# Two products in place of three for the experts' half-filled last tile, and a program whose arms hold the rest of each stretch

## What is computed

```python
for e in range(E):                      # 8 experts
    for k in range(2):                  # first and second choice
        mask = top2[:, k] == e
        h = np.maximum(x[mask] @ w1[e], 0.0)          # 512 -> 1024
        out[mask] += top2_w[mask, k, None] * (h @ w2[e])   # 1024 -> 512
```

## Time and profile before

| what | us |
|---|---|
| median of three runs | 1034.64 (1032.08 to 1034.65) |
| the profiled execution | 1032.71 |
| its span, first to last instruction | 1030.7 |
| TensorE busy in it | 1014.0 (98%) |
| mean granted clock of TensorE | 0.995 of full speed |

### The profile page before, as it was taken

One profiled execution on the slowest core, in us unless ns is written; L12 is line 12 of the kernel. 1 busy time (PEld: TensorE's weight loads), 2 busy tenths in 40 slices (PEclk: granted clock), 3 DMA queues, 4 the chain that ended last, 5 costly groups with the idle time before them and its releaser, 6 DMA issues.

```text
span 1030.7 us, 16726 instructions
## 1 busy us (share of the span) xinstructions
PE 1014.0 (98%) x5934; PEld 932.6 (90%) x5935; DVE 446.0 (43%) x935; ACT 370.1 (36%) x683; POOL 529.8 (51%) x416
## 2 busy tenths in 40 slices
PE   7999999999999999999999999999999999999997
PEld 6999999888989898989898998989898989899895
DVE  6888888773214232433325652222222222222221
ACT  6998988853213132322223413212121212111110
POOL 8698999520000202020202136978788887878752
PEclk8999999999999999999999999999999999999999
DMA  8788886383960101010402175262717163634304
GB/s 175 176 198 200 208 209 164 96 274 116 369 247 1 62 0 62 0 62 0 143 1 73 52 233 167 91 175 71 186 40 212 22 194 71 187 78 140 44 2 51
DMA packets 73986, 124.97 MB, mean 121 GB/s; under 512 B 13377, under 2 KB 30913, under 8 KB 73938
## 3 DMA queue, kind: packets, MB, share of 16 engines
q1 hardware_dynamic: 65218, 104.05, 34.1%
q0 software_dynamic: 8640, 20.00, 9.7%
q10 hardware_dynamic: 80, 0.29, 0.1%
HBM read 78.73 MB, written 36.67 MB: 112 GB/s over the span
## 4 chain that ended last, share of the span: by engine, by line
PE 75%; DVE 1%; issue 0%; POOL 0%; ACT 0%; DVEq 0%; POOLq 0%
PE ps_turn L1714 13%; PE ps_x L1690 10%; PE ps_b L1690 10%; PE ps_x L1779 10%; PE ps_a L1761 9%; PE ps_b L1761 9%; PE ps_small L1714 9%; PE ps_a L1670 2%; PE ps_small L1662 1%; PE ps_turn L1652 1%; PE ps_small L1644 0%; POOL out L1274 0%; PE ps_turn L1802 0%; PE ps_small L1645 0%; DVE y_tile L1455 0%
## 5 line engine op out<-in xcount | busy, mean ns | idle before, releaser
L1217 POOL DMA_INDIRECT expert_rows<-x_rows,slot_idx x36 | 41.7, 1157 | 306.1 <-DVE slot_idx L1590 297.0
L1274 POOL DMA_INDIRECT out<-y_tile,out_rows x40 | 63.2, 1579 | 75.1 <-DVE y_tile L1455 70.9
L1317 ACT CAST xT_high<-ps_a 128x512 fp32r<-128x512 f32 x40 | 23.3, 588 | 188.8 <-PE ps_a L1670 188.8
L1392 ACT COPY prod<-ps_a 128x384 f32<-128x384 f32 x48 | 23.1, 481 | 162.1 <-PE ps_b L1761 162.1
L1597 DVE TENSOR_TENSOR prod<-ps_b,prod 128x384 f32<-128x384 f32 x48 | 26.8, 558 | 123.9 <-ACT prod L1392 123.9
L1690 PE MATMUL ps_b<-xT_high,w_high 128*128 128x256 f32 (+3 forms) x256 | 77.5, 303 | 0.0
L1690 PE MATMUL ps_x<-xT_high,w_high 128*128 128x256 f32 (+3 forms) x256 | 76.9, 300 | 0.0
L1690 PE MATMUL ps_x<-xT_low,w_high 128*128 128x256 f32 (+3 forms) x256 | 76.8, 300 | 0.0
L1690 PE MATMUL ps_x<-xT_high,w_low 128*128 128x256 f32 (+3 forms) x256 | 76.8, 300 | 0.0
L1690 PE MATMUL ps_b<-xT_high,w_low 128*128 128x256 f32 (+3 forms) x256 | 76.8, 300 | 0.0
L1690 PE MATMUL ps_b<-xT_low,w_high 128*128 128x256 f32 (+3 forms) x256 | 76.8, 300 | 0.0
(11 more groups left out here) (272 smaller groups left out, 3011.4 us busy)
## 6 DMA issues: line engine op xcount, KB each, us to landing
spare<-e_w SPq DMA_DIRECT2D x16, 1024.0 KB, 5.3
w_raw<-e_w SPq DMA_DIRECT2D x16, 1024.0 KB, 8.4
expert_rows<-zeros SPq DMA_DIRECT2D x8, 1290.0 KB, 15.9
ex_rows<-expert_rows SPq DMA_DIRECT2D x40, 258.0 KB, 3.9
k_raw<-kT SPq DMA_DIRECT2D x31, 288.0 KB, 4.8
out<-zeros SPq DMA_DIRECT2D x11, 512.0 KB, 10.3
q_raw<-qT SPq DMA_DIRECT2D x16, 288.0 KB, 4.6
q_mix<-q_top SPq DMA_DIRECT2D x16, 288.0 KB, 3.8
```

The costliest lines, as they stand in the source:

```text
L1217: nc.gpsimd.indirect_dma_start(out=rows_dram, out_offset=bass.IndirectOffsetOnAxis(ap=slot_idx[:, k, t:t + 1], axis=0), in_=x_rows[:, t, : ...
L1274: nc.gpsimd.indirect_dma_start(out=out, out_offset=bass.IndirectOffsetOnAxis(ap=out_rows[:, j:j + 1], axis=0), in_=y_tile[j][:], in_offset ...
L1317: nc.scalar.copy(xT_high[:, :, j * P:(j + 1) * P], ps_xT[j % XS][:].rearrange("p (c t) -> p c t", t=P)).then_inc(xhigh, 1)
L1392: nc.scalar.copy(prod[f % 2][:], ps_a[f % 2][:, 0:G]).then_inc(a_copied, 1)
```

## The change

For stretches 1 to 6, and only if the stretch is narrow (at most 576 rows), the fifth tile is made from one combined operand. `hT_last` holds, for the 64 rows, the high half in columns 0 to 63 and the remainder in columns 64 to 127. Products with `ew2_high` and `ew2_low` alone, 16 in all, give two half results in the two halves of the PSUM bank's partitions. Their sum is the result.

- ScalarE (`high_h`) writes the high half into `hT_last` for each unit of the second part, and VectorE (`low_h`) the remainder: one more operation of 64 columns each a unit, in all stretches of the loop, narrow or not.
- `fold_y` on ScalarE copies partitions 64 to 127 of the fifth result to `y_fold` once the fifth tile is there. VectorE's `take_y` for tile 4 waits for that, multiplies it by `is_narrow` (1 or 0, made by GpSimd), adds the lower half, and scales both halves: three operations in place of one, again in all stretches of the loop.
- The three arms are now in the order 640, 608, 576, and in the loop each holds the second products and the transposes too. In the last stretch the arms hold the first product alone, as before, in the new order.

The core of the difference:

```diff
+            def fold_y(g):
+                act.wait_ge(y_done, TILES * g + TILES)
+                act.wait_ge(y_taken, TILES * g)
+                nc.scalar.copy(y_fold[0:HALF], ps_y[(TILES - 1) % YS][HALF:P]).then_inc(y_folded, 1)
...
+                if folds:
+                    dve.wait_ge(y_folded, g)
+                    dve.wait_ge(narrow_known, g + 1)
+                    whole = ps_y[j % YS]
+                    nc.vector.scalar_tensor_tensor(out=y_fold[0:HALF], in0=y_fold[0:HALF], scalar=is_narrow[0:HALF], in1=whole[0:HALF],
+                                                   op0=ALU.mult, op1=ALU.add).then_inc(fold_added, 1)
...
+            def folded_product(g, before, j):
+                pe.wait_ge(y_taken, TILES * before + TILES + j - YS + 1)
+                pe.wait_ge(last_low, FC * before + FC)
+                for f in range(FC):
+                    for rhs in (ew2_high, ew2_low):
+                        mm = nc.tensor.matmul(ps_y[j % YS][:], hT_last[:, f], rhs[:, f], start=(f == 0 and rhs is ew2_high),
+                                              stop=(f == FC - 1 and rhs is ew2_low))
+                mm.then_inc(y_done, 1)
...
-                for k, width in enumerate(WIDTHS):
+                for k, width in reversed([*enumerate(WIDTHS)]):
                     with pe.If(step == k):
                         first_product(g, before, 1, width)
-                pe.wait_ge(weights_cut, 2 * CUTS * before + 2 * CUTS)
-                for j in range(TILES):
-                    second_product(g, before, j)
-                    if not last:
-                        turn_x(g + 1, j)
+                        if not last:
+                            second_products(g, before, False, width == WIDTHS[0])
+                if last:
+                    second_products(g, before, True, False)
```

## The result

| what | before | changed |
|---|---|---|
| median of four runs, us | 1034.43 (1032.08 to 1034.65) | 1093.77 (1091.11 to 1097.42) |
| span of the profiled execution, us | 1030.7 | 1089.2 |
| TensorE busy, us | 1014.0 | 1024.3 |
| mean granted clock | 0.995 | 0.979 |

The ratio is 1.0569 [1.0546, 1.0593]: the changed kernel is 5.7% slower. The forecast of 1037 was wrong, and so was its range, whose end of 1065 is 29 us short; the end of Rival 1, 1067, is 27 us short. The mechanism was Rival 1's, and its prices were too low.

A forecast was written before the change was run, and what follows sets the result against it. TensorE was taken to bound the kernel; -5.6 (products) + 5.3 (first stretch) + 1.5 (last stretch) + 0.5 (loop returns) + 1.0 (clock) = +2.7 us on 1034.6 gave 1037.3, forecast 1037, range 1030.5 to 1065.

The forecast's parts named there:

- Rival 1: TensorE's loop: eight instruction blocks stay, nine are needed, the oldest goes; misses in every pass, 1062 us (1054 to 1067), chance 0.33.
- What bounds the kernel: Expert stage: TensorE, busy 98% of the span, sets the time; work on other engines costs nothing while slack lasts.
- The products saved: Fifth tile on TensorE: eight fewer products in each of three narrow stretches, 24 x 0.2325 us, -5.6 us.
- The side work at no cost: Added ScalarE, VectorE and GpSimd work in the loop's six stretches stays hidden, though the scaled tile comes 2.3 us later.
- Blocks of 256 instructions with starts counted back from 7373: TensorE's program: fetches of 256 instructions, block starts placed by counting back from the last stretch's starving at position 7373.
- The price of a missing block: TensorE jump to a block not asked for: 0.7 us until its fetch begins, 2.4 until it runs, 3.1 us.
- stretch 1: First loop pass, narrow: two missing blocks and two branches less the queue of issued products, +5.3 us (2.9 to 7.7).
- the last stretch: Narrow stretch after the loop: one late block, less the old starving of 0.3 us, +1.5 us (0.3 to 1.8).
- The returns to the loop's top: Ninth block takes the first one's place, so each of five returns misses once: +0.5 us in all (0 to 2).
- the sum: The forecast's main case: -5.6 + 5.3 + 1.5 + 0.5 + 1.0 = +2.7 us, own range 1033 to 1041, chance 0.42.
- The clock: TensorE's granted clock may fall after standing 5 us in the first narrow stretch: +1.0 us (0 to 3).
- Rivals 2 and 3: Far jumps cheap, 1029.0 up to 1031, chance 0.20; late fifth tile holds TensorE in six stretches, 1043 to 1046, chance 0.05.

The follow-up runs named there:

- two shifts: Changed kernel with 168 or 112 do-nothing instructions added ahead of TensorE's loop: 1042.76 us and 1093.49 us.
- the shifted kernel: Changed kernel with 168 do-nothing instructions added ahead of TensorE's loop, which then lies in seven blocks instead of eight: 1042.76 us, ratio 1.0069 to the kernel before.

## Why the prediction was wrong, point by point

- **What bounds the kernel: right.** Every microsecond lost was lost by TensorE, and work added on the other engines was not seen (1.0001 with the side work alone).
- **The products saved, −5.6: right.** 3.77 us for 16 products against 5.58; TensorE's busy time fell by 5.1 to 5.7 us in the two kernels that keep the fold and have short arms.
- **The side work at no cost: right.** The scaled tile comes 2.2 us later where 2.3 was worked out, VectorE's first remainder 1.3 us later, and the cover holds.
- **Blocks of 256 instructions with starts counted back from 7373: right.** This arithmetic foretold which of two shifts, 56 instructions apart, would be 51 us dearer.
- **The price of a missing block, 3.1 us: too small.** It was put together from a fetch that was in flight and one at a block's end. A jump to a block that nobody had asked for took 3.7 to 3.9 us eight times and 4.2 to 4.5 four times, and 4.6 to 5.1 where another fetch is just ahead of its own. So stretch 1 has 7.6 us where 5.3 stood (the upper end of 7.7 held), and the last stretch 2.8 less the old 0.34, that is 2.4, where 1.5 stood, outside its 0.3 to 1.8.
- **The returns to the loop's top, +0.5: this is the step that failed.** It put the ninth block in the first one's place and let the other seven stay. The trace of before could not tell that from eight places of which the oldest is dropped: it showed only that six stay. The runs showed the second. In place of 0.5 us in five passes, every pass fetches every block again (32 + 5 x 9 = 77), and eleven of the thirteen gaps are from this, 38.4 of the 48.8 us. Rival 1 had the mechanism, and its seven places are seven of the eleven: the two pairs at the arms 7.5 us each where 5.3 stood, the three single misses there 2.6 to 2.8 for 2.0, the two pairs at the loop's end 5.6 for 3.1, together 34.4 for 22.8. The other four are the three single returns to the top (1.1 to 1.2 each) and the jump over the last arm at the end of stretch 6 (0.7), which neither the sum nor Rival 1 had: 4.1 us, where the sum had 0.5 for all returns.
- **The clock, +1.0: too small by its kind.** For the one stand of 7.6 us in the shifted kernel it is 2.4 us, and for the thirteen here 14.6 us at the lower level, up to 16 with what is not accounted for. The size taken from the start of the program (four microseconds at half speed, 2 us) was about right for one stand, but Rival 1 had 2 us for all of its stands; the clock fell seven times, 1.5 to 3.1 us each.

- **Rivals 2 and 3: excluded.** Far jumps are not cheap: a gap of 7.6 us where under 1 was the sign. And there is no gap at a fifth unit in any of these kernels; all thirteen stand behind a branch.

The 59.4 us measured are +48.7 idle, −5.4 fold, +14.6 clock and a remainder of 1.5. Had the assumption on the blocks been right, the shifted kernel shows about what would have come out: 7.3 us above its kernel before, where the forecast had 2.7. So the forecast was some 5 us low even in its own case, by the price of a miss and the clock.

The choice itself was poor as well. Rival 1 rested on the plainest way to keep eight blocks, and the sum rested on a way that no row spoke for; "a place fixed by the address" was an argument about how caches are built, and not from the trace. One case with two prices, each too low, made the range end 29 us too early.

## What to carry to other kernels

Before code is put into the arms of a branch within a loop, count the loop of the busiest engine in blocks, with the one fetched ahead: eight stay, nine cost a fetch of every block in every pass, and a few instructions ahead of the loop can decide it. Branch as late and around as little as possible: the same 16 products for 24 gave 5.7% slower in long arms and 0.4 to 0.7% faster with a branch around the fifth tile alone. Price such a jump at 3.7 to 5.1 us a miss, less the depth of the queue of issued work, and add the lowered clock: some 2 us for each stand of 5.6 us and more here.

## What the runs showed of the hardware

- TensorE keeps eight blocks of 256 instructions, the one fetched ahead among them, and drops the oldest: 32 fetches with a loop that needs eight, 32 + 5 x 9 = 77 with one that needs nine. Whether the oldest is the one fetched first or the one used longest ago is open: both give the same fetches in all these programs, and it was not tried.
- In the changed kernel a jump to an absent block took 3.7 to 3.9 us, the fetch starting 0.9 to 1.1 us after the branch, or 4.2 to 4.5 us, the fetch starting 1.9 to 2.2 us after. The block behind the first target was fetched even where the program jumped on at once, 0.4 us ahead of the second target's; the second branch took 4.6 to 5.1 us, and the last of three 5.3 to 5.6 in the kernel with the old order. Why it is 3.7 and not 3.1 is not explained, nor why four fetches start late.
- Instruction-fetch stands have no name of their own in the trace. They are "issue", or are put on the operation that ended last: 1.3 us on VectorE's `hT_low` that went away with an edit of TensorE's program alone.
- The stand of 7.6 us was followed by four microseconds at a granted clock of 0.65 in one kernel and by 5.6 at 0.57 in another. In the changed kernel the lower clock costs 14.6 of the 59.4 us, a quarter.
